# Gated recurrence and two MLP layers on one core: the first tile by halves of the features, the products of low parts last

## What is computed

```python
f = lower_bound + (1.0 - lower_bound) * sigmoid(f_logit)      # (1, 6080, 256)
for t in range(6080):
    h = f[:, t] * h + (1.0 - f[:, t]) * x[:, t]               # a scan over the tokens, per feature
    y[:, t] = h
h1 = y @ w_in                                                 # 256 -> 2048
z = maximum(0.01 * h1, h1) @ w_out                            # 2048 -> 256
h2 = z @ w2_in
g = where(h2 >= 1, h2, where(h2 <= -1, 0.0, (h2 + 1) ** 2 / 4))
out = g @ w2_out
```

## Time and profile before

| | |
|---|---|
| median of three runs | 1010.28 us (1010.21 to 1010.63) |
| the profiled execution | 1009.56 us, its span 1007.4 us |
| PE busy | 995.4 us, 99% of the span |
| DVE, ACT busy | 751.4 and 733.7 us, 75% and 73% |
| POOL busy | 173.7 us, 17% |
| mean granted TensorE clock | 0.992 |
| transfers | 65.45 MB, mean 65 GB/s |

### The profile page before, as it was taken

How to read it: one execution, slowest core, us unless ns; L and a number is a source line. 1 busy time by engine, 2 the same in 40 slices (tenths; PEclk the granted TensorE clock), 3 DMA queues, 4 the chain that set the end, 5 groups by cost and what they waited for, 6 DMA issues and landing times.

```text
span 1007.4 us, 11857 instructions
## 1 busy us (share of the span) xinstructions
PE 995.4 (99%) x4387; PEld 823.5 (82%) x4387; DVE 751.4 (75%) x775; ACT 733.7 (73%) x1015; POOL 173.7 (17%) x179
## 2 busy tenths in 40 slices
PE   8999999999999999999999999999999999999997
PEld 6988788888888888888888878878888887888886
DVE  4667578777777766855578788887888878878786
ACT  5766776767867777766776777787787778678764
POOL 2403144422432310001101101200110110110000
PEclk7999999999999999999999999999999999999999
DMA  7534233244244150054430011110200201110112
GB/s 199 109 71 80 63 94 89 106 98 120 110 103 109 41 152 1 1 178 151 144 119 36 1 42 22 21 43 1 42 15 28 43 0 40 25 18 1 22 21 39
DMA packets 160605, 65.45 MB, mean 65 GB/s; under 512 B 142754, under 2 KB 150052, under 8 KB 160548
## 3 DMA queue, kind: packets, MB, share of 16 engines
q1 hardware_dynamic: 152516, 48.02, 20.1%
q0 software_dynamic: 3584, 15.73, 4.2%
q10 hardware_dynamic: 4448, 0.95, 0.5%
HBM read 40.70 MB, written 23.99 MB: 64 GB/s over the span
## 4 chain that ended last, share of the span: by engine, by line
PE 96%; DVE 1%; ACT 1%; DMA 1%; issue 0%; SPq 0%; DVEq 0%; ACTq 0%
PE S L1099 50%; PE U L1083 41%; PE U L1050 4%; DMA extra<-in_f_logit_dram 1%; PE S L1126 1%; ACT keep L571 0%; DVE VF L845 0%; PE S L1035 0%; DVE H L871 0%; DVE H L884 0%; ACT G L620 0%; DVE V L762 0%; DVE V L756 0%; DVE H L863 0%; DVE G L889 0%
## 5 line engine op out<-in xcount | busy, mean ns | idle before, releaser
L1099 PE MATMUL S<-G,W_down 128*128 128x512 f32 (+2 forms) x2280 | 561.2, 388 | 0.1
L1099 PEld LDWEIGHTS S<-G,W_down 128*128 128x128 f32 x2280 | 427.6, 188 | 86.8 <-ACT sent L630 1.5
L1083 PE MATMUL U<-VF,W_up 128*128 128x512 f32 (+1 forms) x1848 | 461.6, 389 | 1.5 <-DVE H L871 1.2
L1083 PEld LDWEIGHTS U<-VF,W_up 128*128 128x128 f32 x1848 | 345.5, 188 | 77.0 <-issue 3.6
L571 ACT ACTIVATE keep<-U 128x512 f32<-128x512 f32 (+1 forms) x352 | 208.9, 594 | 222.2 <-PE U L1083 222.2
L889 DVE TENSOR_TENSOR G<-H,G 128x1024 fp32r<-128x1024 f32 (+3 forms) x208 | 239.1, 1150 | 101.8 <-ACT G L620 101.1
L620 ACT ACTIVATE G<-H 128x1024 fp32r<-128x1024 f32 (+3 forms) x208 | 200.5, 986 | 6.3 <-DVE H L884 3.5
L884 DVE SCALAR_TENSOR_TENSOR H<-H,extra 128x1024 f32<-128x1024 f32 (+1 forms) x96 | 116.0, 1213 | 46.4 <-ACT extra L598 38.4
L871 DVE TENSOR_TENSOR H<-U,keep 128x1024 f32<-128x1024 f32 (+1 forms) x88 | 107.2, 1218 | 49.8 <-ACT keep L571 49.2
L863 DVE TENSOR_TENSOR H<-U,keep 128x1024 f32<-128x1024 f32 (+1 forms) x88 | 106.7, 1213 | 38.0 <-PE U L1083 35.0
L582 ACT ACTIVATE H<-H 128x1024 f32<-128x1024 f32 x80 | 84.3, 1054 | 0.3 <-DVE H L863 0.3
(11 more groups left out here) (80 smaller groups left out, 393.1 us busy)
## 6 DMA issues: line engine op xcount, KB each, us to landing
ready_up<-G POOLq DMA_DIRECT2D x8, 896.0 KB, 3.9
W_up<-ready_up SPq DMA_DIRECT2D x8, 896.0 KB, 6.3
extra<-in_f_logit_dram SPq DMA_DIRECT2D x44, 128.0 KB, 3.3
extra<-in_x_dram SPq DMA_DIRECT2D x44, 128.0 KB, 3.4
middle<-sent SPq DMA_DIRECT2D x22, 256.0 KB, 2.9
V<-middle SPq DMA_DIRECT2D x5, 1024.0 KB, 5.1
out_dram<-extra SPq DMA_DIRECT2D x40, 128.0 KB, 2.8
ready_down<-G POOLq DMA_DIRECT2D x8, 512.0 KB, 2.9
```

The source lines that it names most:

```text
L1083: mm = nc.tensor.matmul(U[:, bank, 0:w], w_form(j, wp, a), v_form(stage, vp, b), start=fresh and i == 0, stop=i == 2, skip_group_check=True)
L1099: mm = nc.tensor.matmul(S[:, 2 * d + h, 0:w], W_down[:, j, wp, at], g_of(u, e, gp)[:, h * w:(h + 1) * w], start=j == 0 and e == 0 and k == ...
```

## The change

- **First tile by halves of the features.** The tile is loaded as four groups of 112 rows, half 0 and half 1 of the features apart (rows of 512 bytes instead of 1024). Half 0 of `f_logit` comes through two queues, two groups each on SP and ACT. SP no longer waits for data before it starts the weights' loads.
- **Gate beside the drive.** The sigmoid is taken of the negated input, so the drive (DVE) needs only it and `one_less`, and the gate (ACT) runs beside it. A third small number per feature, `less_one`, is computed. ACT does sigmoid and gate of half 0, then of half 1.
- **Weights of pair 0.** POOL writes the high part of its first weights as soon as they land, DVE the low part behind the scans.
- **`first_up`** replaces the two `plain_up` of unit 0: half 0's high passes for both `e`, six transposes of the identity (`COLD3`), half 1's, then the passes with low weights, then those with low data.
- **COLD** is 12, 12 and 6 instead of 16 and 10.
- **Low passes last.** `down_banks` does the two passes on high data for all its banks, and then waits for the low data. In the first unit of a stage the products wait for the high data only, and for the low before the third pass.
- **Scan split** (u = 3, 8, 12): half 0 behind `g_low(u, 0)`, half 1 behind `g_low(u, 1)`.
- **First block unit.** `down` of unit 15 stands whole behind the seven products of u = 16. At u = 1, `plain_up(1, 1)` stands ahead of `down(0, 0)`.

```diff
-COLD1, COLD2 = 16, 10
+COLD1, COLD2, COLD3 = 12, 12, 6
...
-        def load_first(eng, src, dst, done):
+        def load_first(eng, src, dst, k, groups, done):
             by_row = dst.rearrange("p (g d) -> p g d", d=DIM)
...
+            at = slice(k * P, (k + 1) * P)
+            eng.dma_start(by_row[0:GROUP, groups, at],
+                          src[0, groups.start * GROUP:groups.stop * GROUP, at].rearrange("(g p) d -> p g d", p=GROUP)
+                          ).then_inc(done, 16)
...
-            load_first(sp, f_logit, stage_f, s_f0)
+            load_first(sp, f_logit, stage_f, 0, slice(0, 2), s_f0[0])
             sp.dma_start(rows[:, :], lower_bound.rearrange("(k p) -> k p", p=P)).then_inc(s_rows, 16)
-            sp.wait_ge(s_f0, 32)
+            load_first(sp, f_logit, stage_f, 1, slice(0, GROUPS), s_f0[1])
             load_raw(0)
-            sp.wait_ge(s_x0, 32)
             load_raw(1)
...
-            load_first(act, x, stage_x, s_x0)
+            load_first(act, f_logit, stage_f, 0, slice(2, GROUPS), s_f0[0])
+            for k in range(KH):
+                load_first(act, x, stage_x, k, slice(0, GROUPS), s_x0[k])
...
             for k in range(KH):
                 first_sigmoid(k)
-            for k in range(KH):
                 first_gate(k)
-            weights_high(0)
             plain_high(0, 0)
+            down_high(0)
             plain_high(0, 1)
...
+                if fresh:
+                    pe.wait_ge(s_g_high, chunk(u, e))
                 for i in which:
...
+                    one(i, 0)
+                    one(i, 1)
+                if fresh:
+                    pe.wait_ge(s_g, chunk(u, e))
+                for i in which:
+                    one(i, 2).then_inc(s_down, 1)
...
+            def first_up():
...
+                one(0, 0, 0, start=True)
+                one(1, 0, 0, start=True)
+                for i in range(COLD3):
+                    nc.tensor.transpose(U[:, BANK_B, 0:P], ident[:, :], ident[:, :])
+                pe.wait_ge(s_v0_high, 2)
...
-                has_early = u != LAG + 1
+                has_early = u not in (PLAIN, LAG + 1)
...
                 product(u, 6)
+                if u == PLAIN:
+                    down(*early)
                 down(*late)
```

More of the change, by code:

```diff
@@ L306, in load_sums @@
                 if pair < 2:
-                    sp.wait_ge(s_w_up, 6 - pair)
+                    sp.wait_ge(s_w_up, 7 - pair)
                     sp.wait_ge(s_w_down, 7 - pair)
@@ L1033, in transpose_first, with one @@
                 for g in range(GROUPS):
-                    m = min(P, FIRST - g * P)
-                    last = nc.tensor.transpose(S[:, bank + k, g * P:g * P + m], by_row[0:m, g, k * P:(k + 1) * P],
-                                               ident[0:m, 0:m])
+                    last = nc.tensor.transpose(S[:, bank + k, g * GROUP:(g + 1) * GROUP],
+                                               by_row[0:GROUP, g, k * P:(k + 1) * P], ident[0:GROUP, 0:GROUP])
                 last.then_inc(done, 1)
+            def first_up():
+                def one(e, k, i, start=False, stop=False):
+                    wp, vp = PASSES[i]
+                    forms = (A11, A12) if e == 0 else (A21, A22)
+                    return nc.tensor.matmul(U[:, e, 0:FIRST], w_form(0, wp, forms[k]), v_plain(0, vp, k),
+                                            start=start, stop=stop, skip_group_check=True)
+                pe.wait_ge(s_w_first_high, 1)
+                pe.wait_ge(s_v0_high, 1)
+                one(0, 0, 0, start=True)
[3 more added lines that the diff above has]
+                pe.wait_ge(s_v0_high, 2)
+                one(0, 1, 0)
+                one(1, 1, 0)
+                pe.wait_ge(s_w_up, 1)
+                for e in (0, 1):
+                    one(e, 0, 1)
+                    one(e, 1, 1)
+                pe.wait_ge(s_v0, 1)
+                one(0, 0, 2)
+                one(1, 0, 2)
+                pe.wait_ge(s_v0, 2)
+                one(0, 1, 2, stop=True).then_inc(s_plain, 1)
+                one(1, 1, 2, stop=True).then_inc(s_plain, 1)
             def plain_up(u, e):
@@ L1090, in down_banks, with one @@
                 c = 1 - e
+                def one(i, k):
+                    d, h = banks(stage)[i]
+                    wp, gp = PASSES[k]
+                    at = slice(c * DIM + d * P, c * DIM + (d + 1) * P)
+                    return nc.tensor.matmul(S[:, 2 * d + h, 0:w], W_down[:, j, wp, at],
+                                            g_of(u, e, gp)[:, h * w:(h + 1) * w],
+                                            start=j == 0 and e == 0 and k == 0,
+                                            stop=j == PAIRS - 1 and e == 1 and k == 2, skip_group_check=True)
+                if fresh:
+                    pe.wait_ge(s_g_high, chunk(u, e))
                 for i in which:
@@ L1160, in _ @@
             pe.wait_ge(s_bound, 1)
[L1162 removed]
+            first_up()
+            for u in range(1, PLAIN):
                 plain_up(u, 0)
[L1164 to L1171 removed]
+                if u == 1:
+                    plain_up(u, 1)
+                    pe.wait_ge(s_sigmoid, KH)
+                    pe.wait_ge(s_drive, KH)
+                down(u - 1, 0)
+                if u > 1:
+                    plain_up(u, 1)
+                down(u - 1, 1)
             for u in range(PLAIN, UNITS):
```

147 lines of the change are left out of this document (74 added, 73 removed).

## The result

The changed kernel takes 1001.62 us (median; 1001.38 to 1003.27) against 1010.45 us for the kernel before (1010.21 to 1012.71) on the same chip: ratio 0.9908, 95% interval 0.9892 to 0.9923. Two later comparisons on other occasions gave 0.9919 (0.9907 to 0.9931) and 0.9918 (0.9904 to 0.9931), so the gain is 8.2 to 9.3 us by the ratios, where I had forecast 4.7 and a range that ended at 1002.6. Its profiled execution took 1003.27 us, its span 1001.5.

The account below looks back on a forecast made before the run. PE was taken to bound the kernel, busy 995.4 of 1007.4 us. Gains of 4.1 us at the start and 0.6 at unit 16 sum to 4.7 off 1009.56: 1004.9, as median 1005.6, range 1002.6 to 1008.4.

Parts of the forecast that it names:

- The data: At the start: half 0 of f usable at 5.0 us, half 1 of x at 8.5, scan 1 done at 11.2.
- Where the clock goes: PE at the start: clock down at first, back at about 15 us; the start gains 4.1 us; chance 0.35.
- the mark: Point at the start where 18 first products are done: 22.06 us before, forecast 17.9 to 18.0.
- my own two cases (14.3 and 11.8): Start of half 1's products: 14.3 us with PE at the lower clock, 11.8 at the upper, where data decide.
- the forecast case: At the start the clock falls, returns at about 15 us; half 1's products at 14.3; total 1004.9 us profiled, 1005.6 median.
- stays up from the first data on: Rival for the start: upper clock throughout, half 1's products at 11.8, 6.1 us gained there, total 1003.6 us; chance 0.25.
- In-order fillers: At the start eighteen identity transposes and two products stand ahead of half 1's products, delaying them to 14.3 at the lower clock.
- Unit 16: Entry of unit 17: it starts at 106.5 instead of 107.10, 0.6 us gained, bounds 0.2 and 1.0.
- Edits at nothing: Behind the start: low passes last, split scans and alternating banks give nothing, scans perhaps 0 to 0.3 us at unit 16.
- Banks: Rival for second products: about 760 more bank changes, at 10 ns each 7.6 us added, 1013.2; chance 0.05 with other slow-downs.
- The base: Whole kernel: 4.7 us taken off the profiled execution's 1009.56 us, with 0.7 added for the median.

Follow-up runs that it names:

- third: The changed kernel unaltered, timed and profiled again beside the run with only the new start: 1002.39 us.
- apart: The changed kernel with POOL's low part of the second layer's pair 1 one unit later, away from DVE's subtraction in unit 22: 1002.40 us.
- nocold: The changed kernel without any filler transposes of the identity (COLD1, COLD2, COLD3 = 0): 1004.42 us against 1002.29 for the changed kernel on one chip.
- unit16_old: The changed kernel with the old order of unit 16 put back, down of unit 15 in pieces between block products: 1.2 us above the changed kernel.
- start_only: The changed kernel's start with every later edit put back to the old order: 1007.58 us, ratio 0.9968 to the kernel before.
- down_old: The changed kernel with the old order of passes in down and the old waits of the products: 1002.92 us.

## Why the prediction was wrong, by its steps

- **The data: right in kind, too late by about 0.5 to 1 us.** Half 0 of f was in use at 4.14 (forecast 5.0), so there was no idle time ahead of it: its two transfers landed at 3.30 and 3.78, and PE was still in the twelve transposes. My lower end of 4.4 was also summed wrongly: 1.53 + 12 x 0.22 is 4.17. The lag of 1.2 us from the last byte to PE, taken from the last of two long transfers, was too long for a first short one. Half 1 of x landed at 8.0 (8.5) and scan 1 ended at 10.6 (11.2).
- **Where the clock goes: the step that failed.** I wrote that the forecast "takes the clock down at first (twelve transposes ahead of the data instead of sixteen, and pauses between the inputs) and back at about 15". The clock was up from 6.0 us and stayed. Half 1's products started at 11.26 instead of 14.3; of these 3.0 us my own two cases (14.3 and 11.8) put 2.5 on the clock, and the data gave the rest. From there to the mark I had 3.6 us and it took 3.6. So the mark came at 14.83 instead of 18.0, a gain of 7.2 us instead of 4.1. From a fall behind 1.85 us of idle in the old profile I had concluded that pauses of 0.7 us would do the same, and held the gap in front of half 1 of x against the change; the runs show that the clock outlasted gaps of up to 1.46 us in seven profiles and fell with 1.62 (third) and 1.74 us (apart). Apart's profile shows the forecast case happening, its mark 2.7 us behind that of the changed kernel, and nocold puts 2.1 us on the fillers. What decides when the clock first rises is not shown: in unit16_old PE had no gap above 0.2 us from 1.53 on, and it rose only at 10.4.
- **The rival "stays up from the first data on": right in kind, 1.1 us too small.** It had 6.1. Half 1's products were 0.5 us sooner than its 11.8. The rest is DVE: I took 2.22 us for two low passes from the earlier trace rows and let them and the low weights set the mark at 15.3 to 16.5, but one of those two passes had stood beside a POOL instruction. On the new start the two took 1.16 us, the low weights behind them ended at 12.85, and PE waited for neither.
- **A misreading on the way.** I wrote "seven transposes start in 7 to 8 at clock 1.00, five in 9 to 10 at 0.50". The x counts instructions under way, and six and three start. The conclusion stands: at the upper clock they come about twice as fast, and transposes alone had raised it.
- **In-order fillers: right.** The eighteen fillers stand between the data and the products; at the upper clock they cost 1.3 and 0.65 us and fit into the wait for the data, which left PE 0.24 us of wait at 11.26. At the lower clock (apart) the twelve took 2.4 us, and half 1's products started at 13.57, though ACT had their data ready at 11.9.
- **Unit 16: right.** Forecast 0.6 us, with keep behind the weight sums and a wait of 0.4 left: from the first block product of unit 16 to unit 17 it was 8.50 and is 8.00 us, keep stands right behind L515, the wait is 0.36 us. Undoing it cost 0.4 to 0.8 us at that place.
- **"Edits at nothing": the second step that failed.** Undoing the low passes last cost about 0.5 us and undoing the split scans 1.2 us on the new start; neither was run singly on the old one. With unit 16 they make 5.2 us there, and 2.0 us on the old start, where I had 0.6 and at most 0.3 more. I asked whether a wait of PE named DVE there *before*; the question was whether one would once PE came 7 us sooner. Without them most of the gain of the start is lost again: start_only is only 3.2 us below before.
- **Banks: rightly held unlikely.** The second products run at the same pace (0.227 us for 512 columns), and down_old is not faster.
- **The base.** The sum was made against a profiled execution without the 1.51 us wait at unit 22, and the changed kernel's first profile had it. That is why profile against profile gives only 6.3 us where the medians give 8.8. The 0.7 us that I added for the median may stand for the same effect; the runs behind the medians were not profiled.

By place, profile against profile: 7.2 us to the 25th product, 0.3 us (978.1 to 977.8) behind it, 1.5 lost in the wait at unit 22, sum 6.0 of span (5.9 measured); the time outside the span fell by another 0.35 us (2.16 to 1.81). So most of what the forecast missed (4.1 us by the medians) lies in the start (3.1 us).

## What to carry to other kernels

When an engine that bounds everything is moved earlier, every "no wait here" of the old trace has to be asked again: take the new lead off each producer's slack, since what was free at 7 us of lag costs 1.2 to 1.6 us without it. Price the clock from both sides and give the good side its full chance, because one program takes either course from one execution to the next (the changed kernel kept its clock in two profiles and lost it for 3.4 us in the third). Don't take an instruction's price from a row where another engine may have held it up: one low pass was 1.50 us beside POOL and 0.6 us alone. And before comparing two profiles, look for one-off waits in either; here one pair of colliding subtractions is worth 1.5 us.

## What was not expected of the hardware

- Which of two subtractions issued within about 0.4 us comes first decides 1.5 us: DVE's took 2.56 us where POOL's had begun 0.11 us before, and 0.81 us where its own began 0.41 us ahead of POOL's (165.98 in before, 159.34 in down_old).
- The granted clock reads 1.00 ahead of its first recorded change whatever the pace: nocold shows 1.00 in 13 to 14 while its ten products take 3.72 us, the pace of the lower level. In the trace of before the first recorded change is the rise at 4.76, so the 1.00 of the earlier trace rows in 7 to 8 was real, that in 3 to 4 was not: the first sixteen transposes came at 0.21 us each.
- The same start rises to the upper clock at 4.3 to 6.9 us in nine profiles and at 10.4 and 13.3 in two (unit16_old, start_only), with nothing in PE's list ahead of that point that differs.
